# The start of a fused attention and MLP kernel: 1e-9 as an 81st score column, evictions shared by two engines, first mixing in two token parts, other orders

## The reference

```python
# attention, 8 heads of 64: heads 0-3 see the last 32 tokens, heads 4-7 every 4th of the last 128
scores = scale * np.matmul(q, k.transpose(0, 1, 3, 2))
scores = np.where(masks[None, :, :, :], scores, -1000000000.0)
scores = scores - np.max(scores, axis=-1, keepdims=True)
attn = np.exp(scores)
attn = attn / (np.sum(attn, axis=-1, keepdims=True) + 1e-09)
x = np.matmul(attn, v)                       # then (B, S, 512)
# feed-forward with token shift, d_ff 1024
xk = mu_k * x + (1.0 - mu_k) * x_prev
xr = mu_r * x + (1.0 - mu_r) * x_prev
k = np.maximum(xk @ w_k, 0.0)
x = (1.0 / (1.0 + np.exp(-(xr @ w_r)))) * (k * k @ w_v)
# token mixer and channel mixer, d_tok 256, d_ch 1536
h = np.maximum(x.transpose(0, 2, 1) @ w_tok1, 0.0) @ w_tok2
u = x + h.transpose(0, 2, 1)
out = u + np.maximum(u @ w_ch1, 0.0) @ w_ch2
```

## Time and profile before

| | us |
|---|---|
| median of 3 runs | 720.02 (718.41 to 720.12) |
| the profiled execution | 724.47 |
| span of its trace | 722.7 |
| PE busy | 711.4 (98% of the span) |
| DVE, ACT, POOL busy | 383.8, 252.5, 221.8 |
| chain that ended last, PE's share | 94% |

### The profile page before, as it was taken

One profiled execution on the slowest core, in us unless ns is written; L12 is line 12 of the kernel. 1 busy time (PEld: TensorE's weight loads), 2 busy tenths in 40 slices (PEclk: granted clock), 3 DMA queues, 4 the chain that ended last, 5 costly groups with the idle time before them and its releaser, 6 DMA issues.

```text
span 722.7 us, 15625 instructions
## 1 busy us (share of the span) xinstructions
PE 711.4 (98%) x6367; PEld 687.1 (95%) x6367; DVE 383.8 (53%) x657; ACT 252.5 (35%) x620; POOL 221.8 (31%) x233
## 2 busy tenths in 40 slices
PE   8899899999999999999999999999999999999997
PEld 8778899999999999999999999999999999999997
DVE  6377888777686868676853224532245222451222
ACT  3466373544546263536541112311123111231111
POOL 4465684646557475636027000000000000000000
PEclk9899999999999999999999999999999999999999
DMA  9920333223222221042822230303203032010021
GB/s 221 299 49 20 54 75 67 43 51 63 50 52 55 48 53 43 3 100 43 316 99 66 44 64 9 91 10 65 34 11 89 11 64 34 13 21 1 2 34 33
DMA packets 170199, 45.14 MB, mean 62 GB/s; under 512 B 159176, under 2 KB 163728, under 8 KB 170128
## 3 DMA queue, kind: packets, MB, share of 16 engines
q1 hardware_dynamic: 165872, 38.64, 24.8%
q0 software_dynamic: 1088, 4.72, 1.9%
q10 hardware_dynamic: 3168, 0.79, 0.6%
HBM read 29.43 MB, written 4.72 MB: 47 GB/s over the span
## 4 chain that ended last, share of the span: by engine, by line
PE 94%; DVE 3%; ACT 1%; issue 1%; POOL 0%; DVEq 0%; POOLq 0%; ACTq 0%
PE bank L767 12%; PE bank L769 12%; PE bank L768 12%; PE tq L767 8%; PE tq L769 8%; PE tq L768 8%; PE bank L1281 4%; PE bank L1280 4%; PE s L1281 4%; PE bank L1279 4%; PE s L1279 4%; PE s L1280 4%; PE bank L689 3%; PE s L555 2%; PE bank L826 2%; PE bank L653 2%
## 5 line engine op out<-in xcount | busy, mean ns | idle before, releaser
L1256 DVE SCALAR_TENSOR_TENSOR h_lo<-tq,h_hi 128x288 fp32r<-128x288 f32 x48 | 22.0, 458 | 109.6 <-ACT h_hi L1252 109.6
L1256 DVE SCALAR_TENSOR_TENSOR h_lo<-bank,h_hi 128x288 fp32r<-128x288 f32 x48 | 21.9, 457 | 106.1 <-ACT h_hi L1252 106.1
L1252 ACT ACTIVATE h_hi<-tq 128x288 fp32r<-128x288 f32 x48 | 19.8, 412 | 122.3 <-PE tq L769 122.3
L1252 ACT ACTIVATE h_hi<-bank 128x288 fp32r<-128x288 f32 x48 | 19.7, 411 | 121.6 <-PE bank L769 121.6
L854 POOL TENSOR_TENSOR k_lo<-kr,k_hi 128x288 fp32r<-128x288 f32 x64 | 54.5, 856 | 24.3 <-ACT k_hi L850 23.5
L896 DVE RECIPROCAL rg<-rg 128x288 f32<-128x288 f32 x32 | 61.3, 1919 | 0.0
L1281 PE MATMUL bank<-h_lo,C_hi 128*128 128x288 f32 x192 | 57.0, 297 | 0.0
L1280 PE MATMUL bank<-h_hi,C_lo 128*128 128x288 f32 x192 | 56.9, 296 | 0.0
L1050 POOL DMA_DIRECT2D xcur<-X x4 | 3.2, 798 | 174.8 <-DVE U L1198 158.6
L1281 PE MATMUL s<-h_lo,C_hi 128*128 128x288 f32 x192 | 56.8, 296 | 0.0
L1279 PE MATMUL bank<-h_hi,C_hi 128*128 128x288 f32 x192 | 56.8, 296 | 0.0
(11 more groups left out here) (204 smaller groups left out, 2222.3 us busy)
## 6 DMA issues: line engine op xcount, KB each, us to landing
C_raw<-in_moe_w_ch SPq DMA_DIRECT2D x6, 1024.0 KB, 10.9
xcur<-X POOLq DMA_DIRECT2D x4, 1152.0 KB, 5.7
xraw<-xblocks SPq DMA_DIRECT2D x64, 64.0 KB, 2.1
out_x<-blocks SPq DMA_DIRECT2D x112, 36.0 KB, 1.7
vt<-in_v SPq DMA_DIRECT2D x40, 80.0 KB, 2.4
qraw<-in_q SPq DMA_DIRECT2D x128, 24.0 KB, 1.9
kraw<-in_k SPq DMA_DIRECT2D x128, 24.0 KB, 1.9
vt<-in_v SPq DMA_DIRECT2D x7, 320.0 KB, 3.5
```

The source lines that it names most:

```text
L1252: e.activation(hi, ps, ACT.Relu).then_inc(Z.h2h_done, 1)
L1256: e.scalar_tensor_tensor(lo, ps, 0.0, hi.bitcast(F32), ALU.max, ALU.subtract).then_inc(Z.h2l_done, 1)
```

## The change

Seven edits, in the program's order.

1. `sm` has 81 columns for a group, not 80; DVE writes 1e-9 into each 81st column once, with four small memsets at its start. The sum now runs over 81 columns, and the instruction that added 1e-9 (L611) is gone, in all 24 chunks. Mask, exponential and scaling step over that column.
2. For chunks 2 and 3 the second `p_evict` and the second half of `x_evict` are on DVE, and `normalise(3)` is on DVE. Chunk 2's second and chunk 3's first output half go to the scores' banks `s`.
3. The first half's differences and first mixes are done for tokens 0 to 191 and 192 to 287 apart (`first_difference`, `first_mix`).
4. `up` 0 and `up` 1 are interleaved on PE: tiles 0 and 1 for both, then tiles 2 and 3 of each.
5. The prologue's order is new, and it has 23 `keep_warm` multiplications for 37.
6. `split_wk`: the eight `hi` parts are in slots 0 to 3, not 7 to 14; the `lo` parts in slots 9, 8, 10, 9, 11, 10, 12, 11, not 10, 10, 12, 11, 14, 13, 16, 15.
7. The masks are laid out for four groups at a time; the waits that the new banks need are added.

```diff
+KS = KB + 1
+GS = 4 * KS
@@ scores(n)
+                if n == 4:
+                    e.wait_ge(Z.x_done, 4)
+                    e.wait_ge(Z.xv_done, 2)
@@ exponentials(n)
-                e.activation(sb[:, :], sb[:, :], ACT.Exp, scale=0.125).then_inc(Z.e_done, 1)
+                e.activation(groups(sb), groups(sb), ACT.Exp, scale=0.125).then_inc(Z.e_done, 1)
@@ sums(n)
-                e.tensor_reduce(st[:, 8:16], groups(sb), AX.X, ALU.add).then_inc(Z.sum_done, 1)
-                e.wait_ge(Z.sum_done, 2 * n + 1)
-                e.tensor_scalar_add(st[:, 16:24], st[:, 8:16], 1e-9).then_inc(Z.sum_done, 1)
-                e.wait_ge(Z.sum_done, 2 * n + 2)
-                e.reciprocal(st[:, 24:32], st[:, 16:24]).then_inc(Z.rc_done, 1)
+                e.tensor_reduce(st[:, 8:16], sb[:, :].rearrange("p (g x) -> p g x", g=8), AX.X, ALU.add).then_inc(Z.sum_done, 1)
+                e.wait_ge(Z.sum_done, n + 1)
+                e.reciprocal(st[:, 24:32], st[:, 8:16]).then_inc(Z.rc_done, 1)
@@ normalise(n)
+                if n == 3:
+                    e.wait_ge(Z.nm_done, n)
...
+            return dict(vector=gpsimd) if n == 3 else dict(gpsimd=gpsimd)
@@ p_evict(n, h)
+            def vector(e):
+                e.wait_ge(Z.pb_done, n + 1)
+                e.wait_ge(Z.ptb_done, n)
...
+                e.tensor_copy(dst[:, 0], src[:, :, 0:QB])
+                e.tensor_copy(dst[:, 1], src[:, :, 64:TR]).then_inc(Z.ptb_done, 1)
+            return dict(vector=vector) if h and n in (2, 3) else dict(scalar=scalar)
@@ x_evict(n)
-                for s in range(2):
+                for s in range(1 if n in (2, 3) else 2):
...
+                e.tensor_copy(dst, src).then_inc(Z.xv_done, 1)
+            return dict(scalar=scalar, vector=vector) if n in (2, 3) else dict(scalar=scalar)
@@ new
+        def first_difference(d, part):
+            c0, n, done = ((0, SU, Z.difa_done), (SU, HALF - SU, Z.dif_done))[part]
+            def gpsimd(e):
+                if part == 0:
+                    e.wait_ge(Z.x_done, d // 2 + 1)
+                elif d % 2:
+                    e.wait_ge(Z.xv_done, d // 2 + 1)
+                else:
+                    e.wait_ge(Z.x_done, 2 + d // 2 + 1)
+                e.tensor_tensor(dif[:, HALF * d + c0:HALF * d + c0 + n], xcols(0, d, c0 + 1, n), xcols(0, d, c0, n), ALU.subtract)\
+                    .then_inc(done, 1)
...
+        def first_mix(d, part):
...
+                last = e.scalar_tensor_tensor(x0[:, c], dif[:, c], mus[:, d:d + 1], xcols(0, d, c0, n), ALU.mult, ALU.add)
@@ up(hh, f)
-                    for kt in range(DT):
-                        if f == 0:
+                    for g, kt in ([(0, 0), (0, 1), (1, 0), (1, 1), (0, 2), (0, 3)] if f == 0 else [(1, 2), (1, 3)] if f == 1 else
+                                  [(f, kt) for kt in range(DT)]):
@@ prologue()
-                keep_warm(7), transposes(0), keep_warm(4), evictions(0), scores(0), mask_max(0), subtract_max(0),
...
+                keep_warm(7), transposes(0), evictions(0), keep_warm(1), scores(0), mask_max(0), subtract_max(0),
...
@@ feed_forward_all()
-                late[7 + i].append(hi)
-                late[(10, 10, 12, 11, 14, 13, 16, 15)[i]].append(lo)
+                late[i // 2].append(hi)
+                late[(9, 8, 10, 9, 11, 10, 12, 11)[i]].append(lo)
```

More of the change, by code:

```diff
@@ L574, in vector @@
             def vector(e):
-                m0 = KB if j else 3 * KB if dil else 0
+                if j or dil:
+                    m0 = KB if j else 4 * KB
+                    mask = masks[:, m0:m0 + KB].unsqueeze(1).unsqueeze(1).broadcast_to([P, 2, 4, KB])
+                else:
+                    mask = tiles(masks[:, 0:GC], 4).unsqueeze(1).broadcast_to([P, 2, 4, KB])
                 e.wait_ge(Z.s_done, n + 1)
@@ L578, in vector @@
                     e.wait_ge(Z.pb_done, n - 1 if n >= 6 else n - 3)
[L579 to L582, removed]
+                e.tensor_tensor(sb[:, :].rearrange("p (h g x) -> p h g x", h=2, g=4)[:, :, :, 0:KB],
+                                s2[:, :].rearrange("p (h x) -> p h x", h=2)[:, :, 0:GC].rearrange("p h (g x) -> p h g x", g=4),
+                                mask, ALU.add).then_inc(Z.masked, 1)
                 e.wait_ge(Z.masked, n + 1)
@@ L717, in tile, with vector @@
             return t[:, HALF * i:HALF * i + n]
+        def first_difference(d, part):
[5 more added lines that the diff above has]
+                    e.wait_ge(Z.xv_done, d // 2 + 1)
+                else:
+                    e.wait_ge(Z.x_done, 2 + d // 2 + 1)
+                e.tensor_tensor(dif[:, HALF * d + c0:HALF * d + c0 + n], xcols(0, d, c0 + 1, n), xcols(0, d, c0, n), ALU.subtract)\
+                    .then_inc(done, 1)
+            return dict(gpsimd=gpsimd)
+        def first_mix(d, part):
+            c0, n, done = ((0, SU, Z.difa_done), (SU, HALF - SU, Z.dif_done))[part]
+            c = slice(HALF * d + c0, HALF * d + c0 + n)
+            def vector(e):
+                e.wait_ge(Z.mu_done, 1)
+                e.wait_ge(done, d + 1)
+                last = e.scalar_tensor_tensor(x0[:, c], dif[:, c], mus[:, d:d + 1], xcols(0, d, c0, n), ALU.mult, ALU.add)
+                if part:
+                    last.then_inc(Z.xm_done, 1)
+            return dict(vector=vector)
         def difference(hh, d):
@@ L953, in prologue @@
-                difference(0, 0), mix(0, 0, 0), difference(0, 1), mix(0, 0, 1),
-                weighted_values(3), keep_warm(4, tq2, 4), x_evict(3),
-                difference(0, 2), mix(0, 0, 2), difference(0, 3), mix(0, 0, 3)]
+                keep_warm(7), transposes(0), evictions(0), keep_warm(1), scores(0), mask_max(0), subtract_max(0),
+                transposes(1), evictions(1), keep_warm(2), scores(1), mask_max(1), subtract_max(1),
+                transposes(2), evictions(2), exponentials(0), keep_warm(1), scores(2), mask_max(2), subtract_max(2),
@@ new lines, in prologue @@
+                transposes(3), evictions(3), exponentials(1), sums(0), normalise(0), keep_warm(2), scores(3), mask_max(3), subtract_max(3),
+                turn_mu(), exponentials(2), sums(1), normalise(1), keep_warm(4),
+                p_transpose(0, 0), p_transpose(0, 1), p_evict(0, 0), p_evict(0, 1), exponentials(3), sums(2), normalise(2),
+                keep_warm(2), weighted_values(0), sums(3), normalise(3), p_transpose(1, 0), p_transpose(1, 1),
+                x_evict(0), p_evict(1, 0), p_evict(1, 1), first_difference(0, 0), first_difference(1, 0),
@@ L1464, in _ @@
             e.memset(X[:, :].rearrange("p (t n) -> p t n", n=XC)[:, :, 0:1], 0.0).then_inc(Z.zeroed, 1)
+            for t in sm:
+                last = e.memset(t[:, :].rearrange("p (g x) -> p g x", g=8)[:, :, KB:KS], 1e-9)
+            last.then_inc(Z.zeroed, 1)
+            e.wait_ge(Z.zeroed, 4)
             e.wait_ge(Z.const_done, 9)
```

67 lines of the change are left out of this document (44 added, 23 removed).

## The result

| | before | changed kernel |
|---|---|---|
| median | 720.0 us (718.41 to 722.74, 18 runs) | 716.98 us (713.32 to 719.8, 18 runs) |
| profiled execution | 724.47 us | 714.81 us |
| span, mean granted clock | 722.7, 0.992 | 713.0, 1.000 |

The ratio is 0.9954, with an interval of 0.9938 to 0.9971: 0.5% faster, 3.0 us. I had forecast 712.0 us, 8.0 less; 716.98 lies outside the range of 709.0 to 716.3. The two profiled executions are 9.7 us apart, the medians 3.0. That is the thing to explain.

The account below looks back on a forecast made before the run. PE, holding 94% of the chain of waits, was taken to bound the kernel. Prologue -5.9, returning half clock +1.5 and gap at 80 us -3.6 gave -8.0 us: 720.02 to 712.0 us, range 709.0 to 716.3.

Parts of the forecast that it names:

- the prologue's term: Prologue, edits 1 to 5: chunk 4's scores start at 34.4 us against 40.28, -5.9 us with a full clock.
- Walk: Prologue: first product at 27.4 us, three products of 2.03, 0.85 for chunk 4's transposes, so its scores at 34.4.
- I move it by the same amount: Timed median stands 4.45 us below the profiled execution; the profile's saving of 8.0 us is taken off it unchanged.
- the +1.5: Prologue: a half-clock stretch may come again after idle time between identity products; 0 to 2.6 us, taken as +1.5.
- the same distance: Sign to look for: the span's end lies as far from 90 us as before.
- beyond the prologue it is worth nothing: Dropping the 1e-9 addition (L611) shortens DVE's queue, not PE's, so it gains nothing after the prologue.
- rival D: Gaps and clock falls belong to the profiled execution, timed runs have hardly any: 719 us, within 2.2 of 720.0; chance 0.04.
- The gap at 80 us: PE's 2.26 us wait for a probability eviction, and the half clock behind it, go with edit 6's lo parts: -3.6 us.
- ScalarE in slots 0 to 3 at 0: Edit 6's hi copies fill ScalarE in slots 0 to 3 but cost 0, bounds 0 to 1.5 us.
- DMA hidden by 4 us: w_k's last piece lands at 23.2 us and is needed at 27.4, so its loading is hidden by 4 us.
- Scaling 3 on DVE: Prologue: chunk 3's scaling takes 0.8 us on DVE plus 0.5 for POOL's port lock, ending near 22 us.
- The trace of L611: Prologue: L611 took 0.60 us beside POOL's subtraction, read as POOL holding up DVE; basis for adding 0.5 us to scaling 3.

Follow-up runs that it names:

- the held loads: Loads held until chunk 1's probabilities are evicted: in the changed kernel 716.45 us; with w_v first, in the old prologue with the new w_k slots, 716.88 us.

## Why the prediction was wrong

- **The step that failed** is the base of the prologue's term: "Walk: 27.4 + 3 products of 2.03 + 0.85 ... = 34.4, against 40.28: -5.9 us", and with it "I move it by the same amount". The prologue's net term was -5.9 + 1.5 = -4.4 us; measured it was -0.8 (716.53 with edit 6 alone, 715.68 with all edits) and -0.7 (edit 6 undone against before). The walk was good: the changed kernel's profiles have chunk 4's scores at 34.4 to 35.3 where the clock holds. The 40.28 was not: it contained 4.6 us of a slower start, a longer gap and a half-clock stretch, which the same prologue does not have in two later profiles (35.70 with edit 6 alone, 35.18 with the held loads). Against 35.7 the walk would have read 34.4 - 35.7 = -1.3, and the sum -4.9 before any half clock, -3.4 with the +1.5: 716.6, near the 716.98 measured. Part of that nearness is luck: the half clock costs more than 1.5, and edits 1 to 5 and 7 also gain 1.5 us or so behind the prologue, which I had put at nothing ("the same distance", "beyond the prologue it is worth nothing"). The 4.45 us between profile and median, which I carried along as a constant, are about the size of these 4.6. In rival D I named it and gave it 0.04, reasoning that the prologue's gain was queue length; the slots' part proved real (-3.4), the prologue's was mostly D.
- **What comes back in the changed kernel** I had as +1.5, with the idle time between identity products as its cause. It costs about twice that (the median over all 38 runs is 2.8 us above that of the runs at full clock, the gap's own length included), and it has another cause: a wait of TensorE for its instructions inside a block of matmuls. Twelve identity products more did not prevent it (a gap of 1.41 us and a half-clock stretch in their profile).
- **The gap at 80 us**: right in mechanism and size. Predicted -3.6, measured -3.4 alone, and 3.5 when undone. (Of TensorE's waits before I had missed one of 0.53 us at 57.76; it changes nothing in the sum.)
- **ScalarE in slots 0 to 3 at 0**: right; PE has no wait of 0.5 us there in the changed kernel. It is full, though, and passes a late w_v on to PE, as the held loads showed.
- **DMA hidden by 4 us**: right for w_k, and too narrow a question. I checked the landings of data, not what full queues do to the instructions.
- **Scaling 3 on DVE** took 1.03 us for the 0.8 + 0.5 that I had put there, and POOL's scaling ahead of it ended at 21.27 for 20.6. Small. The trace of L611 was a weak witness for that 0.5: L611 reads one tile and a constant, the scaling two tiles.
- Edit 1 (the 81st column) I did not try by itself.

## What to carry to other kernels

Before a saving is subtracted from one profiled execution, ask whether that execution is like the median one: where its time is 0.6% above the median and its mean granted clock below that of the timed runs, the half-clock stretches in it are the first thing to take out of the base, one by one. A faster prologue moves its engines closer to whatever DMA brings, and the instructions are among it: a gap with no semaphore, at the same instruction number in every variant, points to a wait for them, and the trace's packets of the kind "instruction" can confirm it. Holding back loads that are needed some 10 us later, with w_v first, took 1.8 us off here, more than any of the variants of the prologue's own order did.

## What the runs showed of the hardware

- Instructions of TensorE came 0.6 to 2.0 us late at the same matmul number in eight profiles, whose DMA share was 1.0 to 1.4 from 20 to 24 us. The matmul started 1.2 to 1.6 us behind the landing of a 16 KB packet of the kind "instruction". With the share at 0.2 to 0.7 they came in time (two profiles), but once also at 1.1 to 1.2.
- Gaps of 1.41 us and more in that place were followed by a stretch at 0.50 of the clock, some 3 to 7 us long, gaps up to 1.15 us by none. With such a gap and its stretch chunk 4's scores start at 37.05 to 39.14 us, in the new prologue's profiles with a shorter gap at 34.4 to 35.3; three of the four variants with it carry an edit of their own to the prologue, so not all of that is the gap's.
- The timed runs of one kernel can be a mixture of groups up to 4 us apart (714.0 us at a mean clock of 0.999 or more, 718.1 at 0.995 or less), so that two batches of the same kernel gave medians of 715.1 and 717.0.
